# Wider moving operands for small TensorE products, and products of ones ahead of the first tile

## The reference

```python
# 1. linear attention: batch 4, 8 heads, 768 tokens, head size 48
for t in range(S):
    cur = np.einsum('bhd,bhe->bhde', u[None] * kt, vt)
    y[:, :, t] = np.einsum('bhd,bhde->bhe', rt, state + cur)
    state = w[None, :, :, None] * state + np.einsum('bhd,bhe->bhde', kt, vt)
x = y as 3072 rows of 384
# 2. mixture of 8 experts, greedy: all (token, expert) logits in falling order, each token once,
#    each expert at most 384 tokens
logits = x @ w_gate
...
h = np.maximum(x[mask] @ w1[e], 0.0);  out[mask] = h @ w2[e]      # w1 384x1024, w2 1024x384
# 3. the same sizes, every expert sees every token, weighted
logits = x @ w_gate;  P = exp(logits - max), 8 rounds of row and column normalisation
out += P[:, e:e + 1] * (np.maximum(x @ w1[e], 0.0) @ w2[e])
```

## Time and profile before

| | |
|---|---|
| runs shown | 2110.52, 2113.72, 2200.01 us; median 2113.72 |
| profiled execution, its own time | 2112.88 us |
| its span, first to last instruction | 2111.2 us |
| mean granted TensorE clock | 0.974 |
| PE busy, share of the span | 97% |
| DVE, ACT, POOL | 40%, 25%, 17% |

### The profile page before, as it was taken

How to read it: one execution, slowest core, us unless ns; L and a number is a source line. 1 busy time by engine, 2 the same in 40 slices (tenths; PEclk the granted TensorE clock), 3 DMA queues, 4 the chain that set the end, 5 groups by cost and what they waited for, 6 DMA issues and landing times.

```text
span 2111.2 us, 31403 instructions
## 1 busy us (share of the span) xinstructions
PE 2049.4 (97%) x12372; PEld 1877.4 (89%) x12372; DVE 842.6 (40%) x1710; ACT 520.4 (25%) x915; POOL 361.9 (17%) x395
## 2 busy tenths in 40 slices
PE   8984999999999999999999999999999999999998
PEld 7983888899989999899998999989999899998997
DVE  7767777852532323223232232322323223232232
ACT  4540322244221311222122122121311122122121
POOL 8732111265000300030011003000300030012101
PEclk9985988999999999999999999999999999999999
DMA  7721222333000100010001000000100010000000
GB/s 275 238 92 72 100 75 76 110 139 124 1 1 0 60 0 0 0 60 0 0 6 53 0 0 30 30 0 0 60 0 0 0 60 0 0 0 15 27 17 30
DMA packets 18687, 92.33 MB, mean 44 GB/s; under 512 B 2880, under 2 KB 6080, under 8 KB 14528
## 3 DMA queue, kind: packets, MB, share of 16 engines
q1 hardware_dynamic: 13248, 56.85, 7.6%
q0 software_dynamic: 5376, 34.61, 4.5%
HBM read 82.01 MB, written 9.44 MB: 43 GB/s over the span
## 4 chain that ended last, share of the span: by engine, by line
PE 87%; DVE 4%; issue 1%; POOL 1%; DMA 1%; ACT 0%; DVEq 0%; POOLq 0%
PE bank L705 83%; PE bank L802 2%; PE bank L752 1%; PE bank L822 1%; DMA x_in<-x_dram,home 1%; DVE reached L1171 0%; DVE w_lo L1099 0%; DVE slot L1068 0%; POOL x_in L1420 0%; PE bank L808 0%; DVE w_lo L1104 0%; PE bank L745 0%; DVE choice L165 0%; DVE best L145 0%; DVE moved L1189 0%
## 5 line engine op out<-in xcount | busy, mean ns | idle before, releaser
L705 PE MATMUL bank<-x_hi,w_hi 128*128 128x512 f32 (+1 forms) x1344 | 522.2, 389 | 3.0 <-DVE h_lo L1053 3.0
L705 PE MATMUL bank<-x_hi,w_lo 128*128 128x512 f32 (+1 forms) x1344 | 516.2, 384 | 0.0
L705 PE MATMUL bank<-x_lo,w_hi 128*128 128x512 f32 (+1 forms) x1344 | 516.2, 384 | 0.0
L705 PE MATMUL bank<-w_hi,h_hi 128*128 128x384 f32 x1536 | 514.0, 335 | 0.0
L705 PE MATMUL bank<-w_hi,h_lo 128*128 128x384 f32 x1536 | 513.7, 334 | 0.0
L705 PE MATMUL bank<-w_lo,h_hi 128*128 128x384 f32 x1536 | 513.4, 334 | 0.0
L986 ACT ACTIVATE h_hi<-bank 128x512 fp32r<-128x512 f32 x384 | 229.6, 598 | 1128.6 <-PE bank L705 1128.6
L1378 DVE SCALAR_TENSOR_TENSOR h_lo<-bank,h_hi 128x512 fp32r<-128x512 f32 x384 | 265.8, 692 | 547.2 <-ACT h_hi L986 547.2
L705 PEld LDWEIGHTS bank<-x_hi,w_hi 128*128 128x128 f32 x1344 | 254.5, 189 | 48.4 <-issue 3.3
L705 PEld LDWEIGHTS bank<-x_hi,w_lo 128*128 128x128 f32 x1344 | 254.4, 189 | 45.1
L705 PEld LDWEIGHTS bank<-x_lo,w_hi 128*128 128x128 f32 x1344 | 254.5, 189 | 44.0
(11 more groups left out here) (187 smaller groups left out, 1544.4 us busy)
## 6 DMA issues: line engine op xcount, KB each, us to landing
w_raw<-moe_w_dram SPq DMA_DIRECT2D x16, 1536.0 KB, 6.6
rows_in<-rkv_rows_dram SPq DMA_DIRECT2D x24, 576.0 KB, 5.0
rkT<-rk_turned_dram SPq DMA_DIRECT2D x24, 512.0 KB, 3.9
x_dram<-x_rows SPq DMA_DIRECT2D x24, 192.0 KB, 5.0
x_in<-x_dram,home POOLq DMA_INDIRECT x24, 3.3
out_dram<-sums,home POOLq DMA_INDIRECT x24, 2.5
w_raw<-moe_w_dram,w_row POOLq DMA_INDIRECT x16, 7.3
u_tok<-u_rows_dram SPq DMA_DIRECT2D x1, 192.0 KB, 5.0
```

Of the source, the lines that this page charges most:

```text
L705: done = nc.tensor.matmul(out_tile, a, b, start=first and n == 0, stop=last and n == len(terms) - 1, skip_group_check=True)
```

## The change

- Products of scores with v (`y_of`): the moving operand is v's 48 columns twice; the second copy is written to columns 384 to 431 of bank 4, which nobody reads. 8 products in each tile go from 48 to 96 columns.
- First gate: the weights stand in a tile of 128 columns, 8 of weights and 120 of ones that POOL sets once; each product writes 128 columns from the tile's own eight on. Later tiles write their own columns over it.
- Second gate: the same with 96 columns (88 of ones).
- `homes`: the six moving columns are streamed 16 times over, 96 columns in all.
- `count` and `step` stay as they are.
- `keep_busy(n)`: n bf16 products of ones, 512 columns each, into bank 7. 16 stand ahead of the wait for all constants (after the wait for the first three), then 2, 2, 4, 2 around `scores_of(0)` and `scores_of(1)`.
- Two more POOL memsets ahead of its own wait for the constants; the two gate loads write 8 columns into rows of 128 and 96.

```diff
@@ setup
-        gate2 = sb(whole, "gate2", [P, DT, E])
+        gate2 = sb(whole, "gate2", [P, DT, WIDE])
...
-            gate1 = sb(early, "gate1", [P, DT, E])
+            gate1 = sb(early, "gate1", [P, DT, P])
...
-                CONSTS = 8
+                CONSTS = 10
...
-                        sp.dma_start(gate1[:], moe_w_gate).then_inc(gates_loaded, 16)
-                        sp.dma_start(gate2[:], moe2_w_gate).then_inc(gates_loaded, 16)
+                        sp.dma_start(gate1[:, :, 0:E], moe_w_gate).then_inc(gates_loaded, 16)
+                        sp.dma_start(gate2[:, :, 0:E], moe2_w_gate).then_inc(gates_loaded, 16)
...
+                        nc.gpsimd.memset(gate1[:, :, E:P], 1.0).then_inc(const_ready, 1)
+                        nc.gpsimd.memset(gate2[:, :, E:WIDE], 1.0).then_inc(const_ready, 1)
                         pool.wait_ge(const_ready, CONSTS)
@@ tensor, attention
+                        def with_spare(h):
+                            partitions = y_ps.ap[0]
+                            return bass.AP(y_ps.tensor, y_ps.offset + h * D, [partitions, [DM - h * D, 2], [1, D]])
...
-                                    last = nc.tensor.matmul(y_ps[:, h * D:(h + 1) * D], scores[:, t % 2, h % 2, q],
-                                                            rows_in[:, t % SLOTS, 2, h * D:(h + 1) * D],
+                                    last = nc.tensor.matmul(with_spare(h), scores[:, t % 2, h % 2, q],
+                                                            rows_in[:, t % SLOTS, 2, h * D:(h + 1) * D].unsqueeze(1).to_broadcast([P, 2, D]),
...
-                                last = nc.tensor.matmul(logit_ps[:, t * E:(t + 1) * E], xT[:, t % 2, d], gate1[:, d],
+                                last = nc.tensor.matmul(logit_ps[:, t * E:t * E + P], xT[:, t % 2, d], gate1[:, d],
...
+                        def keep_busy(n):
+                            for _ in range(n):
+                                nc.tensor.matmul(banks[7][:].rearrange("p (a b) -> p a b", b=P), ones_bf[:],
+                                                 ones_bf[:].unsqueeze(1).to_broadcast([P, 4, P]), start=True, stop=True,
+                                                 skip_group_check=True)
+
+                        pe.wait_ge(const_ready, 3)
+                        keep_busy(16)
                         pe.wait_ge(const_ready, CONSTS)
...
                         for t in range(T):
+                            if t < 2:
+                                keep_busy(2 + 2 * t)
                             scores_of(t)
+                            if t < 2:
+                                keep_busy(2)
@@ tensor, choice
-                            last = nc.tensor.matmul(logits2_ps[:, j * E:(j + 1) * E],
+                            last = nc.tensor.matmul(logits2_wide[:, j * E:j * E + WIDE],
                                                     x2T[:, d, CAP * s + j * P:CAP * s + (j + 1) * P], gate2[:, d],
...
-                            last = nc.tensor.matmul(home_ps, is_place[:, :, t], token_at[:, :, :, t].rearrange("p a s -> p (a s)"),
+                            tokens = token_at[:, :, :, t].rearrange("p a s -> p (a s)")
+                            last = nc.tensor.matmul(home_wide.rearrange("p (c n) -> p c n", c=HOME_COPIES), is_place[:, :, t],
+                                                    tokens.unsqueeze(1).to_broadcast([P, HOME_COPIES, 2 * CT]),
                                                     start=(t == 0), stop=(t == T - 1))
```

More of the change, by code:

```diff
@@ L91, in attention_moe_kernel @@
     PLACE_PARTS = 4
+    HOME_COPIES = 16
+    WIDE = 96
     SLOTS = 6
@@ L233, in attention_moe_kernel @@
                 xT_ps = banks[6][:, 0:DM]
-                logit_ps = banks[7][:, 0:T * E]
+                logit_ps = banks[7]
                 table_ps = banks[6]
@@ L648, in attention_moe_kernel @@
             count_ps, moved_ps, tally_ps = banks[3][0:NJ, 0:E], banks[3][:, E:2 * E], banks[3][:, 2 * E:3 * E]
-            logits2_ps = banks[4][:, CAP:CAP + CT * E]
+            logits2_ps, logits2_wide = banks[4][:, CAP:CAP + CT * E], banks[4][:, CAP:]
             ties_ps = banks[7][:, 0:1]
             ranks_ps = banks[7][:, 4:6]
-            home_ps = banks[7][:, 8:8 + 2 * CT]
+            home_ps, home_wide = banks[7][:, 8:8 + 2 * CT], banks[7][:, 8:8 + HOME_COPIES * 2 * CT]
             cleared, places_made = sem(late, "cleared"), sem(late, "places_made")
```

## The result

The changed kernel takes **2129.87 us** (median of 5 runs, 2128.62 to 2130.68), the kernel before 2114.15 us beside it. The ratio is 1.0075 [1.0064, 1.0087]: 16 us slower, less than the 2% that were called "same", but outside the forecast range and on the other side of the time before. The profiled execution takes 2130.68 us; its span is 2129.0 us against 2111.2 us.

What follows compares the result with a forecast made beforehand. PE, busy at full clock from 363.65 us on, is untouched; only the first 364 us, with PE partly at half clock, can gain. Terms +1.1, +0.2, -9.2, -3.7, -2.1 give -13.7 us from 2112.88: 2099.2 us, range 2093 to 2108.

Steps and rivals of the forecast that it cites:

- Widening as such: All widened products: stationary loads hide the extra columns; `y_of` 0 us, first gate +1.1 us, `homes` and second gate +0.2 us.
- The falls of the clock: Phases 2 to 5: wide `homes` and gates keep columns streaming, so the clock stays up as in phase 6; -9.2 us.
- The end of the attention: `y_of(23)`, the gates behind it and the turn: the clock holds until the work ends; -3.7 us.
- The start: Tiles 0 and 1: products of ones warm the array, `outer_of(2)` starts earlier, bounded by POOL's keys at 20.04 us; -2.1 us.
- Rival C: Start: the clock drops in the pause ahead of the table, +2 in place of -2.1 us; 2103.3 us, chance 0.12.
- The gate and the products with v: Attention: first gate costs 0.05 us for each of 22 gates, +1.1 us (ends 0 and 2.2); products with v cost 0.
- The second gate: Phases: wide columns hide under the stationary loads; counted together with `homes` at +0.2 us.
- D: Attention: the two-piece product with v halves the stream, 20.4 us on the path; 2119.6 us, chance 0.05.
- A: Whole kernel: the clock follows PE's being busy, not columns, so only the products of ones act; 2112.1 us, chance 0.08.
- B: Phases: half the falls stay, as counts stay narrow; 4.6 of the 9.2 us kept, 2103.8 us, chance 0.14.
- The long stretch: Half-clock stretch from 151 to 217 us, phases 0 and 1: left as it is, 0 us, ends -1.5 and +1.5.

Runs made afterwards that it cites:

- e2: Changed kernel with the six moving columns of `homes` stored side by side, still streamed as 96 columns: 2108.01 us, ratio 0.9973 to the kernel before.
- e1: Changed kernel with `homes` narrow again at 6 columns, all other edits kept: 2109.72 us, ratio 0.9979 to the kernel before.
- e9: Changed kernel with the six moving columns of `homes` 16 bytes apart, still 96 wide: 2128.86 us, one run.
- e10: Kernel before with `homes` alone changed to 96 strided columns, 48 bytes apart: 2134.41 us, ratio 1.0104.
- e7: Kernel before with `homes` alone changed to 96 packed columns: 2107.31 us, ratio 0.9974.
- e8: e2 with v wide only in the last three tiles, first gate in the last four, second gate narrow: 2100.78 us, ratio 0.9942 to the kernel before.
- e11: The same kernel as e2 on another chip: 2104.11 us, ratio 0.9964 to the kernel before.
- e6: Changed kernel with the six moving columns of `homes` 4 bytes apart, still 96 wide: 2101.86 us, one run.
- e12: Kernel before with only the products with v and the first gate widened, no products of ones: 2108.01 us, ratio 0.9991.
- e4: Kernel before with the products of ones (`keep_busy`) alone, nothing widened: 2110.20 us, ratio 0.9987.
- e3: Changed kernel with 4 copies in `homes` and not 16, 24 strided columns: 2108.97 us, ratio 0.9987 to the kernel before.
- e5: Changed kernel with 8 copies in `homes` and not 16, 48 strided columns: 2105.42 us, a single run.

## Why the prediction was wrong, by its own steps

**The step that failed** is in "Widening as such": "a quarter of that, for 96 columns, is 47 ns and hides under 73", with +0.2 us for `homes` and the second gate. The 189 ns for 384 columns were read from products whose columns lie side by side, and were carried to an operand whose columns lie 48 bytes apart. Those products differ from `homes` in data type too (float32 in the view, not bf16), but that did not matter: packed, 96 bf16 columns do hide, at 70 ns a product (e2). The rows of before could not show the price, for six such columns hide in the same 70 ns. Against e1, `homes` cost 2.4 us in each of seven groups and 2.1 us in phase 1, 18.8 us in all, and clock on top. At half clock the step looked for 0.3 us in phase 1, where the whole 2.2 us is on the path; for packed columns its figure of 86 ns was near (80 ns between starts in phase 1 of e2).

**The falls of the clock** (-9.2 us): the mechanism held, but the change did not carry it out. Strided, the products bring columns to the array too slowly, and the clock falls at each `homes` of phases 2 to 6 (the changed kernel, e9, e10: five falls each). Packed (e2, e7, e8, e11) or at a step of 4 bytes (e6) there is no fall in the phases. With `homes` narrow, or 24 or 48 strided columns wide, there are one to four: four in before, three in e12, two in e4, one in e1, e3 and e5. It is not a matter of the one execution that was profiled: all 12 of e11 have a mean granted clock of 0.981 to 0.984, the kernel before beside them 0.973 to 0.979.

The size was taken from one execution, and that one has more falls than most: its mean clock is 0.974, and the kernel before beside e1 and e2 has 0.974 to 0.982, with a median of 0.980. From `choice` of phase 2 to that of phase 6 before takes 172.97 us, e11 161.64 us, 11.3 us less, and e2 167.49 us, 5.5 us less. The two lie on either side of the forecast. Beside executions with narrow `homes` on the same chip the gain is smaller: e2 against 168.9 us in e1, e11 against 166.6 us in e12.

What had not been foreseen is a fall behind the phases (6.8 us at 419.0 us in e11, 3.4 us in e7 and e8), where before has none: from the sixth to the seventh `turn` e11 takes 37.36 us, before 34.52 us, so 2.8 us are given back. It is of another kind. In every execution PE waits there for 2.9 to 3.0 us, for DVE's `h_lo`, and in ten of the fourteen a fall begins in this wait or within 1.3 us of its end. e4, which widens nothing, has it, and e2, e6, e12 and before do not.

**The end of the attention** (-3.7 us): right, -3.4 us from tile 23's scores to the last gate, in the changed kernel and in e12.

**The start** (-2.1 us): right at the place named, `outer_of(2)` 1.93 us earlier, with POOL's keys ending at 19.78 us, close to the bound of 20.04 us; the view puts the last wait down to DVE's state, which the prediction did not name. But 0.6 us of it is lost on the way to tile 23 even with narrow products (115.7 us from tile 2's scores to tile 23's in e4 and e8, 115.1 us before). Rival C happened once in ten profiled executions with products of ones, in e1.

**The gate and the products with v** (+1.1 and 0): both mis-sized. In an ordinary tile the gate takes 0.79 and not 0.73 us, and the last four products with v pass on 0.04 us (0.44 us to the gate behind them, 89.72 to 90.16, where four narrow ones take 0.40 us): 0.10 us a tile, 2.0 us in e12. That lies inside the bound of 2.2 us, but at its far end. With the 0.6 us above it makes up the 2.6 us of the table. e8, which widens only where the clock was about to fall, pays little of it.

**The second gate**: its six products take 0.73 us to the count behind them and not 0.66 us (263.15 to 263.88; before 260.35 to 261.01). Twelve such groups make 0.8 us, where the +0.2 us had to do for `homes` too. e8 keeps it narrow and loses no clock in the phases; the packed `homes` is enough there.

**The rivals.** D had the right kind of mechanism, the form of the moving operand setting the pace, and 20 us as its price, and named the wrong product: the two-piece product with v, whose columns lie side by side, stays at 111 ns a record. The forecast's error was to look for a new form among the operands that the change rewrote, and not at the one it only repeated. A is refuted for the phases by e2, e6 and e7, in which PE is as busy and the clock stays up. The idle-gap rule of the Trainium skill (TensorE: Matmul & The Clock Gate, section "Why this matters for your kernels") does not account for the falls in the phases: e10's fall is filled to 6.80 of 6.80 us, and the remedy was columns, not fewer gaps. The fall behind the phases, at a wait of 2.9 to 3.0 us, does fit it. B, half the falls staying, is not what the packed kernels show within the phases.

**What the sum would have been.** With `homes` packed the forecast of -13.7 us stands against -5.7 us and -7.6 us, by the ratios of e2 and e11. 2.0 + 0.8 + 0.6 us of the shortfall are the terms above, less the 1.3 us already in the sum, and 2.8 us the new fall in e11; the kernel before spans 2108.2 to 2119.5 us in the runs beside e1 and e2, so which execution's falls one starts from is worth as much as the rest. The long stretch, left at 0 with ends of 1.5 us, was also too narrow: the clock rises at 214.40 us in e2 and at 207.42 us in e11, and phase 2 takes 43.2 and 39.7 us. Part of that, and of the phases 3 and 4 at 41.4 us each in e2 and 40.6 us in e11 with no fall in either, has a place in the trace: DVE reads one count of each phase late (`full`, L1200).

```profile
278.49 0.15 DVE L1200 TENSOR_TENSOR full<-bank,room 16x8 bf16<-16x8 f32 x1 [1.76 <-PE bank L823]
```

```profile
272.58 0.15 DVE L1200 TENSOR_TENSOR full<-bank,room 16x8 bf16<-16x8 f32 x1 [0.88 <-PE bank L823]
```

The first row is e2's and the second e11's, the same search of phase 3: 0.9 us and 0.1 us behind the end of the count. e1, e3 and e4, which ran on e2's chip, have this delay too, and the eight others, on two other chips, do not. It goes with the chip and not with the kernel. **Open** stays what holds DVE there.

## What to carry to other kernels

Before a moving operand is widened or repeated, look at the distance between its neighbouring columns in memory: a price that does not show at 6 or 24 columns comes out at 48. Lay out the operand so that its columns are packed where it is written once and read many times; here that turned a loss of 0.8% into a gain of 0.3% (with `homes` left at six columns the gain was 0.2%). Then widen only where the trace shows the clock falling, for the wide form costs a little wherever the clock is up anyway. And before a gain is sized from one profiled execution, see whether it is a typical one: the mean clock of several executions tells that.

## What the runs showed of the hardware

- A bf16 moving operand whose columns lie 16 or 48 bytes apart is read at some 1.7 to 1.9 ns a column (96 columns in 180 and 175 ns, 48 in 92 ns); at 4 bytes, or side by side, 96 columns take the 70 ns a product that six take.
- That pace does not follow TensorE's granted clock: 4.37 us for the group at 0.50 (phase 1), 4.36 us where part of it ran at 1.00 (phase 2), 4.38 us where all of it did (at 450.14 us, behind the phases).
- Reading the same 12 bytes 16 times over (a step of 0) costs nothing: the group takes 1.67 us in e2 and 1.69 us in e1, where they are read once.
- In the phases the granted clock fell to 0.50 (1.2 GHz) with PE called busy for the whole of the fall (6.80 of 6.80 us in e10), at products that stream few columns or stream them slowly. Behind the phases it fell at an idle time of PE of 2.9 to 3.0 us, in ten of fourteen executions.
